# Exponentials ahead of copies, masks ahead of normalising, and output products ahead of turned tiles in a fused attention, expert and gated-MLP kernel

## What is computed

```python
# attention: 8 heads of 64
scores = scale * q @ k.T
thresh = max(scores, -1) - tau
scores = where(scores >= thresh, scores, -1e9)
attn = softmax(scores)              # + 1e-9 in the denominator
x = attn @ v                        # heads side by side: (4, 576, 512)

# experts: 8, one for each token; a sticky gate can keep the expert of the token before
e = argmax(x @ w_gate)              # or the last token's e
out = softmax(x @ w_gate)[e] * (relu(x @ w1[e]) @ w2[e])

# gated MLP with a product over the positions
h = gelu(x @ w_in); u, v = halves of h
v_n = layernorm(v) * g_ln
gated = u * (w_sg @ v_n + b_sg)
y = x + gated @ w_out
```

## Time and profile before

| what | value |
|---|---|
| median of three runs | 971.12 us |
| lowest and highest | 968.65 and 971.57 us |
| the profiled execution, whole | 971.14 us |
| its span, first to last instruction | 969.3 us |
| PE busy | 915.3 us, 94% of the span |
| DVE busy | 557.6 us, 58% |
| ACT busy | 415.4 us, 43% |
| POOL busy | 378.1 us, 39% |
| mean granted TensorE clock | 0.984 of full speed |

### The profile page before, as it was taken

The page is one execution under the profiler, slowest core; times in us unless marked ns, Lnnn a source line. Parts: engine busy times, 40 slices in busy tenths (PEclk is TensorE's granted clock), DMA queues, the critical chain, the costliest instruction groups (busy, mean ns, idle before and its releaser), DMA issues.

```text
span 969.3 us, 16335 instructions
## 1 busy us (share of the span) xinstructions
PE 915.3 (94%) x6071; PEld 772.3 (80%) x6071; DVE 557.6 (58%) x1208; ACT 415.4 (43%) x793; POOL 378.1 (39%) x344
## 2 busy tenths in 40 slices
PE   7899998999899998999999999999999999999996
PEld 6777887788778877788888887788869788897884
DVE  6777777777776745817854688460035445344352
ACT  4767666666666633333333333333323132031220
POOL 4344435544574241455655565554214023040100
PEclk7999999999999999999999999999999999999998
DMA  6322332232223014735655466430030020200101
GB/s 150 75 62 75 86 85 64 63 111 62 63 74 111 14 51 158 230 107 145 203 171 186 139 204 209 151 103 19 1 110 2 1 98 1 95 3 1 50 1 49
DMA packets 47709, 86.82 MB, mean 90 GB/s; under 512 B 8076, under 2 KB 16396, under 8 KB 47632
## 3 DMA queue, kind: packets, MB, share of 16 engines
q1 hardware_dynamic: 43632, 76.32, 26.6%
q0 software_dynamic: 4000, 9.45, 3.0%
HBM read 73.42 MB, written 15.99 MB: 92 GB/s over the span
## 4 chain that ended last, share of the span: by engine, by line
PE 52%; DVE 5%; DMA 3%; issue 1%; ACT 1%; DVEq 0%; POOLq 0%
PE ps_y L1432 4%; PE ps_y L1434 4%; PE ps_y L1433 4%; PE ps_a L1704 4%; PE ps_a L1706 4%; PE ps_a L1705 4%; PE ps_h L1393 4%; PE ps_h L1395 4%; PE ps_h L1394 4%; PE ps_v L1704 3%; DMA w_raw<-in_w 2%; DVE w_low L1326 2%; PE ps_v L1706 2%; PE ps_v L1705 2%; PE ps_r L1704 2%; PE ps_r L1705 2%
## 5 line engine op out<-in xcount | busy, mean ns | idle before, releaser
L822 DVE SCALAR_TENSOR_TENSOR probs<-ps_s,floor,expd 128x576 f32<-128x576 f32 x144 | 117.0, 812 | 61.6 <-ACT expd L469 61.1
L512 ACT COPY probs_t<-ps_ring 128x512 f32<-128x512 f32 (+1 forms) x192 | 105.9, 560 | 102.4 <-PE ps_ring L606 93.4
L558 PE MATMUL ps_s<-k_high,q_split 128*128 128x288 f32 x336 | 107.6, 338 | 13.3 <-DVE probs L822 10.0
L1318 DVE CAST w_high<-w_raw 128x1024 fp32r<-128x1024 f32 (+1 forms) x63 | 65.4, 1053 | 89.1 <-PE ps_h L1395 44.1
L469 ACT ACTIVATE expd<-ps_s,max_tau 128x576 f32<-128x576 f32 x144 | 108.0, 750 | 5.1 <-DVE max_tau L808 5.1
L808 DVE TENSOR_REDUCE max_tau<-ps_s 128x1 f32<-128x576 f32 x144 | 106.7, 741 | 0.3 <-PE ps_s L559 0.3
L637 PE MATMUL ps_ring<-probs_t,v_pair 128*64 128x144 f32 x1280 | 93.9, 295 | 3.6 <-ACT probs_t L512 3.6
L559 PE MATMUL ps_s<-k_low,q_split 128*128 128x288 f32 x336 | 93.0, 299 | 0.0
L558 PEld LDWEIGHTS ps_s<-k_high,q_split 128*128 128x128 f32 x336 | 65.0, 193 | 34.6 <-DVE probs L822 24.2
L1326 DVE TENSOR_TENSOR w_low<-w_raw,w_high 128x1024 fp32r<-128x1024 f32 x66 | 88.9, 1367 | 3.2 <-POOL ids L1192 3.2
L637 PEld LDWEIGHTS ps_ring<-probs_t,v_pair 128*64 128x64 f32 x1280 | 77.2, 139 | 14.7 <-ACT probs_t L512 7.1
(11 more groups left out here) (263 smaller groups left out, 2054.4 us busy)
## 6 DMA issues: line engine op xcount, KB each, us to landing
w_raw<-in_w SPq DMA_DIRECT2D x63, 512.0 KB, 4.1
k_in<-in_k SPq DMA_DIRECT2D x30, 288.0 KB, 4.2
q_in<-in_q SPq DMA_DIRECT2D x30, 288.0 KB, 4.2
v_pair<-in_v SPq DMA_DIRECT2D x16, 256.0 KB, 2.7
x_rows_dram<-scratch SPq DMA_DIRECT2D x4, 1024.0 KB, 4.6
out<-scratch SPq DMA_DIRECT2D x4, 1024.0 KB, 4.3
scratch<-in_dense SPq DMA_DIRECT2D x8, 384.0 KB, 5.5
scratch<-y_rows_dram SPq DMA_DIRECT2D x3, 1024.0 KB, 5.5
```

The source lines that it names most:

```text
L558: nc.tensor.matmul(out, lhs, k_high[par][:, h, cols], start=first, stop=False)
L822: nc.vector.scalar_tensor_tensor(out=row_of(pair, w).rearrange("p (a c) -> p a c", a=2), in0=scores(n), scalar=floor[:, n % 4:n % 4 + 1], ...
```

## The change

Five edits, in three places.

1. ACT, attention: in each step the exponential of unit n is issued ahead of the copies of the step's items, not behind them.
2. DVE, attention: in each step the mask of unit n-1 is issued ahead of the normalising of the value product.
3. PE and DVE, gated MLP: the output products of the first two tiles of rows come straight behind the product over positions. Then four tiles of the next batch are turned, then the output products of tiles 2 and 3, then the fifth tile is turned, then the last output product. DVE's `y_low` moves in the same way.
4. PE, gated MLP: the products of tiles 0 and 1 wait at each of their four chunks c only for the pieces of `gated_low` that they read (2c+1 of the batch's eight); the others wait for all eight.
5. SP: in the last batch each of the five tiles is stored with a DMA of its own as soon as its row sum is out.

```diff
--- before.py
+++ after.py
@@ -533,11 +533,11 @@
 
         for n in steps:
             pair, w = unit_of(n)
+            if n < UNITS:
+                exp_scores(n)
             for k, item in enumerate(STEPS[n]):
                 if item[0] not in BY_DVE:
                     evacuate(FIRST_OF_STEP[n] + k, item)
-            if n < UNITS:
-                exp_scores(n)
             for h in range(2):
                 if w == SCALE_AT[h] and pair + 1 < ALL_PAIRS:
                     scale_q(pair + 1, h)
@@ -974,12 +974,12 @@
             pair, w = unit_of(n)
             if n < UNITS:
                 row_max(n)
+            if 0 < n <= UNITS:
+                mask(n - 1)
             if n > 0:
                 for k, item in enumerate(STEPS[n - 1]):
                     if item[0] == "pv":
                         pv_normalise(FIRST_OF_STEP[n - 1] + k, item)
-            if 0 < n <= UNITS:
-                mask(n - 1)
             if n < UNITS:
                 row_floor(n)
             if w == 1 and 0 < pair <= ALL_PAIRS:
@@ -1535,6 +1535,12 @@
 
         def body(b, par, k, last):
 
+            if last:
+                for t in range(QT):
+                    sp.wait_ge(row_out, QT * b + t + 1)
+                    sp.dma_start(batch_rows(io["out"], b, P * t, rows(t)), y[par][0:rows(t), t, :]).then_inc(stored, 16)
+                sp.wait_ge(stored, 32 * b + 16 * QT)
+                return
             sp.wait_ge(row_out, QT * b + QT)
             sp.sem_inc(passed, 1)
             sp.dma_start(batch_rows(io["out"], b, 0, FULL * P).rearrange("(t p) d -> p t d", p=P), y[par][:, 0:FULL, :]).then_inc(stored, 16)
@@ -1660,10 +1666,12 @@
                 dve.wait_ge(a_out, A_ITEMS * b + QT + i + 1)
                 nc.vector.tensor_tensor(u_t[:, c, cols], spatial[:, half, :], u_t[:, c, cols], ALU.mult).then_inc(gated, 1)
             gated_low(b, V_ITEMS - 1)
-            if not last:
-                y_low(b + 1)
             for t in range(QT):
                 r = rows(t)
+                if not last and t == 2:
+                    y_low(b + 1, range(4))
+                if not last and t == 4:
+                    y_low(b + 1, range(4, QT))
                 dve.wait_ge(row_done, QT * b + t + 1)
                 nc.vector.tensor_tensor(y[par][0:r, t, :], ps_r[0:r, t % 2, :], y[par][0:r, t, :], ALU.add).then_inc(row_out, 1)
 
@@ -1714,8 +1722,8 @@
                 last = nc.tensor.transpose(y_bank(b, t)[:, c * r:c * r + r], y[par][0:r, t, P * c:P * c + P], ident[0:r, 0:r])
             last.then_inc(y_done, 1)
 
-        def turn_y(b, par):
-            for t in range(QT):
+        def turn_tiles(b, par, tiles):
+            for t in tiles:
 
                 if t < 2:
                     pe.wait_ge(a_out, A_ITEMS * b)
@@ -1769,16 +1777,19 @@
                         last = product(ps_v[:, half, 0:HALF], lambda p: v_parts[p][0:r, t, P * c:P * c + P],
                                        lambda p: w_sg[p][0:r, t, HALF * half:HALF * half + HALF], t == 0, t == QT - 1)
                     last.then_inc(mixed, 1)
-            if not last_batch:
-                turn_y(b + 1, 1 - par)
             for t in range(QT):
+                if not last_batch and t == 2:
+                    turn_tiles(b + 1, 1 - par, range(4))
+                if not last_batch and t == 4:
+                    turn_tiles(b + 1, 1 - par, range(4, QT))
                 r = rows(t)
-                if t == 0:
+                pe.wait_ge(row_out, QT * b if t < 2 else QT * b + t - 1)
+                if t >= 2:
                     pe.wait_ge(gated_split, V_ITEMS * b + V_ITEMS)
-                    pe.wait_ge(row_out, QT * b)
-                elif t >= 2:
-                    pe.wait_ge(row_out, QT * b + t - 1)
                 for c in range(DC):
+                    if t < 2:
+                        pe.wait_ge(gated_split, V_ITEMS * b + 2 * c + 1)
+                        pe.sem_inc(passed, 1)
                     last = product(ps_r[0:r, t % 2, :], lambda p: gated_parts[p][:, c, P * t:P * t + r],
                                    lambda p: w_out[p][:, c, :], c == 0, c == DC - 1)
                 last.then_inc(row_done, 1)
```

## The result

| | before | after |
|---|---|---|
| median | 969.98 us (4 runs, 968.65 to 971.57) | 946.10 us (4 runs, 944.84 to 947.40) |
| profiled execution, whole and span | 971.14 and 969.3 us | 944.84 and 943.0 us |
| mean granted clock | 0.984 | 0.991 |

The ratio is 0.9753, with a 95% interval of 0.973 to 0.9777: 23.9 us of the medians.

A forecast was written before the change was run, and what follows sets the result against it. PE was taken as the bound nearly everywhere, so gains lie only in its idle or lower-clock time. 6.0 - 0.5 + 1.0 + 2.5 + 3.6 + 2.3 + 1.7 + 1.9 = 18.5 us off 971.1 gave 952.6 us, range 947 to 960.

The forecast's parts named there:

- 0.20 of every wait is no stall: Attention after 40 us, PE's score load waiting for masks: 16.2 - 49 x 0.20 = 6.4 us, taken as 6.0 (3 to 6.4).
- the ring: Attention, PE's waits for ACT's copies: step 4's 0.68 us stays; a tie at step 2 loses 0.5 us (0 to 3.8).
- the waits for DVE's table: Attention: two waits of PE, 1.8 us together, behind masks that waited for an exponential; 1.0 us gained (0 to 1.4).
- The start: Start of attention, before step 14: DVE's chain sets the pace; 2.5 us gained (0 to 6.6).
- move as a block: Experts' stretch, PE 98.6% busy: expected to move as a whole, with 0 us gained.
- The MLP and the clock: Gated MLP: 3.6 us at three batch ends, 2.3 in the last batch, 1.7 from no lower clock behind it.
- The last store: End of kernel: 128 KB store lands 2.8 us after issue, as the 144 KB load did; 1.9 us gained.
- That attention gives nothing: Rival, attention: score waits return as longer waits for copies; only the end's 9.5 us left, 961.6 us; chance 0.13.
- the five stores queue: Rival, end of kernel: each store's completion stands behind the one before; 1.9 us lost, 954.5 us; chance 0.10.
- That the start gives nothing: Rival, start: a DMA holds the exponentials, and the clock falls again in the MLP; 956.8 us; chance 0.10.
- The slower rival: Attention: masks waiting for late exponentials delay normalising, and PE waits for the ring bank; 30 us lost, 992 us; chance 0.03.
- L606 and L637 keep their 0.68 and 0.24: Attention, sign of being right: PE's waits for copies at steps 4 and 2 stay at 0.68 and 0.24 us.

The follow-up runs named there:

- both moves: Changed kernel with q scaled in steps 0 and 1, and the exponentials of steps 2 and 4 behind the copies PE waits for: 942.33 us, ratio 0.9723.
- the experiment: Edits 3 and 4 alone, against the kernel before, with attention and stores as before: 962.69 us, ratio 0.9938.
- the best: As the kernel with both moves, but normalising ahead of the mask in the step behind the routing scan: 938.70 us, ratio 0.9696.
- two exponentials moved: Changed kernel with the exponential behind the tails' copy in step 2 and behind the copies of sums and rest in step 4: 945.19 us, ratio 0.9728.

## Why the prediction was too small

It named the right edits, places and signs, and was 6.5 us off. 1.1 of that is its base, 971.12, since the median that came out for the kernel before is 969.98. The gain was 23.9 us where the sum has 18.5, and most of the 5.4 missing lie in attention (12.9 in the profile, 9.0 in the sum). That the time came within 0.9 us of the range is in part luck: two terms of attention were wrong in opposite directions.

**The step that failed: "0.20 of every wait is no stall".** I took 49 x 0.20 = 9.8 us off the 16.2 us of PE's waits for masks, since the same load shows gaps of 0.20 us where nothing holds it. Of those 35 gaps 33 stand behind value products. Of the 49 waits 44 stand behind transposes, and there the load has no gap if the mask is ready. So nothing was to be taken off: the row fell from 16.2 us to 3.9, by 12.3 where the term says 6.4, and of the 18 waits left 17 stand behind value products, 0.2 us each. The kernel before shows both, in PE's timeline:

```profile
94.03 0.60 PE L606 MATMUL ps_ring<-ident,probs 128*128 128x128 f32 x4
94.61 0.40 PE L558 MATMUL ps_s<-k_high,q_split 128*128 128x288 f32 x1
...
97.41 0.38 PE L558 MATMUL ps_s<-k_high,q_split 128*128 128x288 f32 x1
```

From the transposes at 94.03 to the scores are 0.58 us, and so it is, or longer, in each of the four steps of a plain pair in which the load waited behind transposes; from those at 97.00 to the scores at 97.41 only 0.41, because at 97.00 PE came late itself and the mask was there. The changed kernel has 0.35 in the four (88.01 to 88.36, in the rows of its PE above), and still 0.41 in the fifth.

In the four places of a plain pair that had a wait, 0.58, 0.58, 0.96 and 0.69 became 0.35: 0.23 + 0.23 + 0.61 + 0.34 = 1.4 us a pair. The row at 97.41 was within my reach, and I read only the one at 101.52.

**The second term, the ring, was wrong the other way.** I said that L606 at step 4 "stays" at 0.68 us, and took 0.5 us for the tie at step 2. PE now comes to both places earlier, at a chain of ACT that is no shorter, so the waits became 0.92 and 0.38, 0.38 us a pair. From unit 17 to unit 143 the two rows grew by 3.3 us (L606 from 7.8 to 9.5, L637 from 3.3 to 5.0), where I took 0.5. The copy that is waited for does not move when the waiting engine speeds up; a wait that "stays" has to be worked out from the releaser's time, and not from the waiter's. Net, a plain pair went from 19.72 to 18.61 us, 1.1, as 1.4 - 0.4 says, to within rounding. The third term, the waits for DVE's table, came as said: both are gone, with 1.3 us of PE's idle time, where I took 1.0.

**Pairs with routing gave some back.** From the mask of unit 17 to that of unit 143, 14 pairs at 1.1 us would have been 15.5 us; it was 10.4 (forecast 6.0 - 0.5 + 1.0 = 6.5). The three plain pairs gained 3.3, the other eleven 7.0. One pair in each batch even became longer, 22.65 us instead of 22.00. One pair with a scan on DVE takes 22.2 us with edits 1 and 2 and 20.3 with edit 1 alone. The scan is 3.67 us long in the one and 1.33 in the other (the last section has the reason), and the mask stands ahead of the normalising in the one only. The order explains 0.4 us of it: of the two kernels with both moves, the one with the mask first takes 22.0 us in this pair, the one with the normalising first 21.6, and both have a scan of 2.6 us. How much the scan itself costs no run here separates, since the length of the scan and that of the pair don't go together: the kernel before has a scan of 1.85 us and takes 23.35. I had bounded the loss ("some of them stand beside routing work", 3 to 6.4), but not seen it in a row. At the last mask 14.7 us were gained, at the last value product 12.9. The 1.8 us between are no new wait: the masks now come earlier against PE's work, and between the last mask and the last value product PE has 194 matmuls where it had 179.

**The start** gave 4.3 us up to unit 17 (its mask at 43.76 instead of 48.10), 3.0 up to unit 10 (29.88 instead of 32.89), against 2.5 forecast from DVE's own work of 1.6 us a unit. The mechanism was right: from unit 3 to unit 10 pass 10.85 us, 1.55 a unit. But the size is that of one execution. The second execution of the changed kernel reached unit 17 at 45.02, edits 1 and 2 alone at 44.25, so the gain is 3.1 to 4.3 us. The lower clock does not explain the spread by itself: it lasts 10.2, 13.7 and, in the first execution, 6.8 us there.

**The experts** "move as a block": false for this pair of executions, by 3.3 us, and not by the change, as far as the other profiles tell. Some 2.8 us of the kernel before were waits for `w_low`, which the changed kernel had in one execution (1.4) and not in the other.

**The MLP and the clock**: 7.8 us measured in the profile, 7.6 forecast as 3.6 + 2.3 + 1.7; 6.9 by the experiment. The profiles bear out the larger figure: without a low stretch at the MLP's entry it takes 253.4 us in the old order (edits 1 and 2, edit 1 alone) and 245.7 in the new, 7.7 apart; with one there, 255.0 and 247.3. All kernels with the old order have a low stretch behind the wait of 2.3 us in the last batch, those with edits 3 and 4 have none there, and edit 3 alone has four. By its sum and by the MLP's entry such a stretch costs 1.5 to 1.6 us, against 1.7 in the forecast.

**The last store**: 2.4 us measured in the profile and 2.1 by edit 5 alone, against 1.9 by the row of the 144 KB load. In the trace the last store lands 2.26 us after its issue (940.37 to 942.63), in edit 5 alone 2.25, where the load's row gave 2.8; the span ends 0.4 us behind the landing, as it did before (968.93 and 969.33). The Trainium skill, "DMA: Bandwidth & Descriptors", section "Anatomy of one DMA", gave 2.3 us for the store and 2.4 gained, by an estimate from its figures, and the trace agrees with it more closely; the section is on DMAs that GpSimd issues, while these are issued by SyncE. The rule of the Trainium skill, same page, section "Rules for kernel authors", to coalesce many small transfers does not carry over to this end of a kernel: with pieces of 256 and 128 KB the coalesced form, the one of before, is the slower by 2.1 us.

**The rivals.** That attention gives nothing fell by the experiments with edits 1 and 2 together and with edit 1 alone, that the five stores queue by the landing in 2.0 us. That the start gives nothing fell too: edit 1 alone reaches unit 17 at 45.32 instead of 48.10, so it is ACT's order that held the exponentials there, and no low stretch stands behind the end of a batch of the MLP. The slower rival described a mechanism that exists: with edit 2 alone it makes the kernel 6.9 us slower. It needs the late exponentials, which edit 1 removes, and it acted in the pairs with routing, 9.0 us in all with over half in two of them, not in "some 60 value products", so that its price of 30 us was over three times too high. In the list of what would show it, DVE's waits, the load's waits, the fifth tile, the clock of the last batch and the last store came as said; "L606 and L637 keep their 0.68 and 0.24" did not. Of the signs of being wrong none came in full: L637's wait grew to 0.38 us in a plain pair, and PE's wait for L847 at the routing step is 1.47 us where it was 1.38.

The three parts add up by medians to 12.3 + 6.9 + 2.1 = 21.3 us, by ratios to 10.3 + 6.0 + 3.0 = 19.3, against 23.9 for all five edits. The intervals (4.9, 2.9 and 1.7 us to either side) are together wider than the difference, so whether the parts help each other is not shown.

## What to carry to other kernels

Before taking a fixed part off each wait as "no stall", look for the same pair of instructions at a place where the awaited result was ready, behind the same kind of predecessor; the gap left there is the allowance, and it may be none. When a change lets an engine come sooner, work out every later wait anew from its releaser, because a wait that another engine's chain ends grows by what was gained. Work that stood ahead of a result was its cover: move it away only together with finer waits.

## What the runs showed of the hardware that I had not expected

**DVE and POOL hold each other up.** The same scan on DVE takes 1.33 us with edit 1 alone, 1.85 in the kernel before and 3.67 in the changed one. What differs beside it is when POOL's TENSOR_TENSOR starts. The changed kernel, POOL and DVE:

```profile
153.28 2.65 POOL L406 TENSOR_TENSOR q_split<-q_in,q_split 64x1152 fp32r<-64x1152 f32 x1
153.46 3.67 DVE L904 TENSOR_TENSOR_SCAN scratch<-scratch 8x576 f32<-8x576 f32 x1
```

and with edit 1 alone:

```profile
158.59 1.33 DVE L904 TENSOR_TENSOR_SCAN scratch<-scratch 8x576 f32<-8x576 f32 x1
158.71 3.66 POOL L406 TENSOR_TENSOR q_split<-q_in,q_split 64x1152 fp32r<-64x1152 f32 x1
```

Whichever starts 0.1 to 0.2 us later is longer by the rest of the other: 153.28 + 2.65 + 1.2 = 157.13, the end of the scan. In the kernel before POOL's row ends at 163.92 and the scan, begun at 163.27, at 165.12, again 1.2 us later. No wait is shown; the row is simply long. The Trainium skill, "SBUF — State Buffer", section "SBUF: two separate sides", tells of such a lock, held for the whole instruction, between a DVE instruction with two SBUF inputs and a GpSimd one that reads SBUF; the trace agrees, with these four rows. It is seen in the rows, not made by an experiment that moves the one instruction alone.

**The experts' waits for `w_low` seem to go with the same thing.** In the kernel before a `w_low` of the experts is three times as long as the usual 1.22 us beside POOL's work:

```profile
568.93 4.06 DVE L1326 TENSOR_TENSOR w_low<-w_raw,w_high 128x1024 fp32r<-128x1024 f32 x1
569.34 2.55 POOL L1215 TENSOR_TENSOR hidden_t_low<-scratch,hidden_t_high 128x512 fp32r<-128x512 f32 x2
```

Here the order of the starts does not fit: `w_low` starts 0.41 us ahead of POOL's rows, which keep their usual 1.3 us each, and it is still `w_low` that is long. Why, the rows don't show. Between 550 and 620 us, the eleven profiles in which PE waited for `w_low` have at least two such lengthened rows or pairs of rows each, the three without that wait (the first of the changed kernel, the one with both moves, and the best) at most one. That speaks for the same hold-up as the cause, and does not prove it. What decides in one execution who comes first was not tested, and stays open.

**The clock.** Outside the start, the granted clock fell to the lower level in thirteen places behind waits of PE of 2.0 to 2.4 us: five last batches in the old order, four batches with edit 3 alone, and two routing steps each in the kernel with edit 2 alone and in the one with the two exponentials moved. Behind the waits of 1.2 to 1.5 us at the ends of batches and at the routing steps of the kernels before and after it did not fall. But the length alone does not decide. At the MLP's entry PE waits 1.3 to 1.5 us in all fourteen profiles, and in five of them (before, the changed kernel's first, edit 2 alone, two exponentials moved, both moves) the clock falls 1.6 to 2.5 us after it, in the other nine not. (There are further low stretches at the end of attention, whose cause I did not look for.) And the kernel with both moves waited 1.96 and 1.91 us and kept the full clock,

```profile
156.53 0.66 PE L670 MATMUL ps_ring<-ident,x_t 128*128 128x128 f32 x4 [1.96 <-DVE scratch L855]
```

```profile
157.00:160.00 3.00, 3.00 (x36) 1.00 0.19 39
241.50:245.00 3.50, 3.50 (x39) 1.00 0.15 31
```

while waits of 2.00 and 2.02 us at the same place, above, brought 0.54 and 0.50. A stretch of 3.4 us at the lower clock costs 1.5 to 1.6 us, by the sums above, some two thirds of the wait ahead of it.
